# The opening of a one-core attention and two-MLP kernel: first state sums behind the first product, first outputs ahead of the second scores, few wide dummy products for many small ones

## The chip, the cores and the metric

The kernel runs on one core of a Trainium2 chip. The core has five engines with an instruction stream each: PE (TensorE, matmul), DVE (VectorE), ACT (ScalarE), POOL (GpSimd) and SP (SyncE, which here only issues DMAs). They meet through semaphores. The metric is the device time of one execution in microseconds, the median of three runs. PE has two clock levels, 1.2 and 2.4 GHz; the profile writes them as a granted clock of 0.50 and 1.00.

## The reference, cut to what matters

```
# attention, B=4 H=8 S=768 D=48, a state of D x D per head:
y[t]  = r[t] . (state + (u*k[t]) v[t]^T)
state = w[t][:, None] * state + k[t] v[t]^T
# x = y as 3072 tokens x 384, then two MLPs
h = x @ w_in (384 x 2048);  x = (h * clip(h+3,0,6)/6) @ w_out
x = x / rms(x) * rms_g;     out = (silu(x @ w_gate) * (x @ w_val)) @ w_out2   (384 x 1536)
```

All inputs and outputs are float32.

## The kernel before

The sequence is cut into groups of 64 steps of two batches each; 24 groups `g` in all, groups 0 and 1 being the first 64 steps of the two pairs of batches. For a group, DVE scans the decays (`prep_scan`, tile `cum`), takes four reciprocals (`prep_inv`) and multiplies by the keys (`prep_k`, tile `ki`); POOL multiplies `r` by the decays (`prep_r`, tile `rd`) and, for groups 0 and 1 alone, `r` by `k` (`rk_mul`, tile `xo`). PE then forms the scores (`scores`), the transposed keys (`keys`), the state sums (`sums`) and the outputs (`outputs`, whose parts are `inside` and `inside3`), and for groups 0 and 1 the bonus term (`bonuses`). ACT puts the bonus on the diagonal (`fill_bonus`), copies the transposed keys (`copy_keys`, tile `kiT`) and rounds the outputs to the MLP's input (`x1_hi`, tile `xs`); DVE masks the scores (`mask_scores`), subtracts the rounded part (`x1_lo`) and takes the sums into the state (`update_state`).

The first MLP follows tile by tile, `e` = 0 to 6. Tile 0 is half a tile (256 tokens) and is made of groups 0 and 1; while it runs, groups 2 and 3 are worked in between. For each slice `f` of 16, PE makes the hidden product `up(e, f)` (three products per 128 rows, from a rounded weight and its rest), ACT and DVE apply the gate (`up_gate`, `hidden`), and PE adds the slice into the output, `down(e, f-2)`. In tile 0 the weights are still on their way: SP and ACT load them (`load_up`, `load_dn`), ACT rounds them (`split_up`), and POOL subtracts (also `split_up`). PE's `up(0, f)` waits for POOL's part.

Nothing is scheduled by a program: the order of each engine is the order in which its code is written, and each engine waits in order. What stands ahead of the first product of tile 0 is the opening, about 22 us. In it PE also runs dummy products on a tile of ones (`busy`, L1278), 20 + 3 + 3 + 4 of them, 128 columns each. A float32 matmul stands in the trace as two matmul records and two weight loads, so a dummy is four instructions.

## Time and profile before

| | us |
|---|---|
| median of 3 runs | 932.94 (931.34 to 935.17) |
| the profiled execution, its own time | 935.66 |
| its span | 933.9 |
| PE busy | 921.6 (99%) |
| DVE, ACT, POOL busy | 521.3, 361.7, 291.9 |

The span is what the trace covers; 1.8 us of the execution lie around it. PE is busy in nearly all of it, so the time is the sum of PE's work and of the few places where PE waits. Most of these lie in the opening. The trace's chain of waits goes back from the last instruction to what released each step; its pieces called "issue" are time in which an engine waited for nothing that the profile shows.

### The profile page before, as it was taken

What the parts mean: (1) busy time and instruction counts of PE and PEld (TensorE: products, weight loads), DVE (VectorE), ACT (ScalarE), POOL (GpSimd) and SP (SyncE); (2) the same over time, 40 slices, a digit from 0 to 9 for tenths busy, and PEclk for the clock granted to TensorE, in tenths of its full rate; (3) what the DMA queues carried; (4) which work ended last, traced back from release to release, by engine and by line L of the source; (5) the groups of instructions that cost most, each with busy time, mean ns of one, the idle gap of its engine ahead of it and who ended that gap; (6) DMA issues with size and microseconds to landing.
All of it is one profiled execution on the core that took longest, in us unless ns stands there. A gap on an engine that the chain in (4) does not pass through costs nothing.

```text
span 933.9 us, 17547 instructions
## 1 busy us (share of the span) xinstructions
PE 921.6 (99%) x7064; PEld 772.9 (83%) x7064; DVE 521.3 (56%) x752; ACT 361.7 (39%) x786; POOL 291.9 (31%) x244
## 2 busy tenths in 40 slices
PE   7999999999999999999999999999999999999998
PEld 7899988888888888888888888888888888888886
DVE  6888976566666666315774553553463373363332
ACT  4557454354444445336463123223223223223212
POOL 4789544454454444324351011011011001101000
PEclk9999999999999999999999999999999999999999
DMA  9874442233223231014221010010000001000000
GB/s 255 237 208 129 109 131 60 63 105 86 75 61 107 69 83 51 22 39 135 86 83 45 0 35 34 1 34 34 0 34 35 1 19 50 0 1 34 1 1 34
DMA packets 33008, 60.40 MB, mean 65 GB/s; under 512 B 6112, under 2 KB 19936, under 8 KB 32928
## 3 DMA queue, kind: packets, MB, share of 16 engines
q1 hardware_dynamic: 27104, 50.82, 18.7%
q10 hardware_dynamic: 5824, 8.47, 3.1%
q8 instruction: 56, 0.92, 0.4%
q14 instruction: 24, 0.20, 0.1%
HBM read 47.66 MB, written 9.44 MB: 61 GB/s over the span
## 4 chain that ended last, share of the span: by engine, by line
PE 93%; DVE 4%; issue 1%; DMA 1%; ACT 1%; SPq 1%; DVEq 0%; ACTq 0%
PE acc L1079 34%; PE bank L1050 11%; PE bank L1052 11%; PE bank L1051 11%; PE pair L1050 5%; PE pair L1051 5%; PE pair L1052 5%; DVE ki L731 1%; PE acc L1113 1%; PE pair L1132 1%; PE pair L1189 1%; PE pair L1161 1%; DVE cum L719 1%; PE bank L1068 1%; PE bank L1153 1%
## 5 line engine op out<-in xcount | busy, mean ns | idle before, releaser
L1079 PE MATMUL acc<-gs,w_dn 128*128 128x512 f32 (+1 forms) x1512 | 357.0, 382 | 1.2 <-issue 1.2
L1079 PEld LDWEIGHTS acc<-gs,w_dn 128*128 128x128 f32 x1512 | 272.9, 188 | 55.1 <-issue 1.3
L945 POOL TENSOR_TENSOR gs<-act_g,gs 128x512 fp32r<-128x512 f32 (+1 forms) x96 | 122.1, 1272 | 208.3 <-ACT gs L550 208.2
L1050 PE MATMUL bank<-xs,w_up 128*128 128x512 f32 (+1 forms) x459 | 171.9, 374 | 1.4 <-DVE state L762 1.2
L1052 PE MATMUL bank<-xs,w_up 128*128 128x512 f32 (+1 forms) x459 | 169.1, 368 | 0.0
L1051 PE MATMUL bank<-xs,w_up 128*128 128x512 f32 (+1 forms) x459 | 169.0, 368 | 0.0
L801 DVE SCALAR_TENSOR_TENSOR act_g<-act_u,bank 128x512 f32<-128x512 f32 (+1 forms) x112 | 67.5, 603 | 139.8 <-ACT act_u L542 139.8
L869 DVE TENSOR_TENSOR act_u<-act_u,bank 128x512 f32<-128x512 f32 x72 | 49.5, 688 | 146.8 <-ACT act_u L612 146.8
L542 ACT ACTIVATE act_u<-bank,half 128x512 f32<-128x512 f32 (+1 forms) x112 | 70.0, 625 | 150.8 <-PE bank L1052 139.9
L616 ACT ACTIVATE gs<-act_g 128x512 fp32r<-128x512 f32 x72 | 45.5, 632 | 155.9 <-DVE act_g L875 155.9
L1050 PEld LDWEIGHTS bank<-xs,w_up 128*128 128x128 f32 x459 | 86.4, 188 | 18.0 <-DVE state L762 1.6
L612 ACT ACTIVATE act_u<-bank 128x512 f32<-128x512 f32 x72 | 43.1, 598 | 149.0 <-PE bank L1052 149.0
L1051 PEld LDWEIGHTS bank<-xs,w_up 128*128 128x128 f32 x459 | 86.5, 188 | 14.8
L1052 PEld LDWEIGHTS bank<-xs,w_up 128*128 128x128 f32 x459 | 86.4, 188 | 14.6
L991 POOL TENSOR_TENSOR xs<-ntmp,xs 128x512 fp32r<-128x512 f32 x18 | 26.1, 1448 | 225.8 <-ACT xs L575 225.8
L731 DVE RECIPROCAL ki<-cum 112x128 f32<-112x128 f32 x96 | 84.2, 921 | 0.8
L550 ACT ACTIVATE gs<-act_g 128x512 fp32r<-128x512 f32 (+1 forms) x96 | 57.2, 596 | 69.4 <-DVE act_g L801 67.8
L875 DVE TENSOR_TENSOR act_g<-act_u,pair 128x512 f32<-128x512 f32 x72 | 49.5, 688 | 52.0 <-PE pair L1052 51.3
L879 DVE TENSOR_TENSOR gs<-act_g,gs 128x512 fp32r<-128x512 f32 x72 | 55.3, 768 | 36.8 <-ACT gs L616 36.3
L1050 PE MATMUL pair<-xs,w_up 128*128 128x512 f32 x144 | 56.0, 389 | 0.0
L1051 PE MATMUL pair<-xs,w_up 128*128 128x512 f32 x144 | 56.0, 389 | 0.0
L1052 PE MATMUL pair<-xs,w_up 128*128 128x512 f32 x144 | 56.0, 389 | 0.0
(121 smaller groups left out, 1121.6 us busy)
## 6 DMA issues: line engine op xcount, KB each, us to landing
rkn<-in_rkN SPq DMA_DIRECT2D x22, 384.0 KB, 4.1
rkt<-in_rkT SPq DMA_DIRECT2D x44, 192.0 KB, 3.6
val<-in_valN SPq DMA_DIRECT2D x22, 256.0 KB, 3.0
x<-x_dram SPq DMA_DIRECT2D x6, 768.0 KB, 4.2
dec<-in_decT SPq DMA_DIRECT2D x46, 97.5 KB, 2.3
x_dram<-xo SPq DMA_DIRECT2D x5, 768.0 KB, 4.1
out<-xo SPq DMA_DIRECT2D x5, 768.0 KB, 3.3
raw_dn<-in_w_out SPq DMA_DIRECT2D x14, 192.0 KB, 4.8
```

What stands on the lines that cost most here:

```text
L542: act.activation(act_u[:, f % 2, tok], ps_h[f % 2][:, tok], ACT.Relu, scale=1.0 / 6.0, bias=half[:, 0:1]).then_inc(s_u, 1)
L550: act.activation(gs[:, f % GRING, 0, tok], act_g[:, f % 2, tok], ACT.Copy).then_inc(s_ghi, 1)
L731: dve.reciprocal(ki[0:DP, q, p, :, :], cum[0:DP, q, p, :, 1:T1]).then_inc(s_inv, 1)
L801: dve.scalar_tensor_tensor(out=g_of(e, f), in0=act_u[:, f % 2, tok], scalar=1.0, in1=ps_h[f % 2][:, tok], op0=ALU.min, op1=ALU.mult).then_ ...
L869: dve.tensor_tensor(act_u[:, f % 2, :], act_u[:, f % 2, :], ps_h[f % 2][:, :], ALU.mult).then_inc(s_silu, 1)
L875: dve.tensor_tensor(act_g[:, f % 2, :], act_u[:, f % 2, :], ps_v[f % 2][:, :], ALU.mult).then_inc(s_h, 1)
L879: dve.tensor_tensor(gs[:, f % GRING, 1, :], act_g[:, f % 2, :], gs[:, f % GRING, 0, :].bitcast(F32), ALU.subtract).then_inc(s_hlo, 1)
L945: pool.tensor_tensor(gs[:, f % GRING, 1, tok], act_g[:, f % 2, tok], gs[:, f % GRING, 0, tok].bitcast(F32), ALU.subtract).then_inc(s_glo, 1)
L1050: pe.matmul(dst, w_hi, x_hi, start=first, stop=False)
L1051: pe.matmul(dst, w_hi, x_lo, start=False, stop=False)
L1052: last = pe.matmul(dst, w_lo, x_hi, start=False, stop=end)
L1079: last = pe.matmul(ps_o[m][:, tok], w[:, wp, m * P:(m + 1) * P], gs[:, f % GRING, xp, tok], start=f == 0 and a == 0, stop=f == nf - 1 and ...
```

## The change

- PE: `sums(0)` moves from ahead of `scores(1)` to behind the first hidden product `up(0, 0)`. `keys(1)` moves to behind `up(0, 2)`, into bank 7. `outputs(0)` now precedes `scores(1)`. The dummies become 4 + 1 + 2 of 512 columns.
- DVE: of group 1's reciprocals the last, and its `prep_k`, come behind `mask_scores(0)`. `update_state(0)` comes behind `hidden(0, 0)`.
- POOL: the wait for both scans stands ahead of `prep_r(0)` instead of `rk_mul(1)`.
- ACT: the fourth `load_up` and the two `load_dn` leave it for SP; `split_up(0)` and both `place_val3` come ahead of group 1's bonus; `keep_last` comes behind `x1_hi(1)`; `copy_keys(1)` comes behind `up_gate(0, 3)`.
- SP: group 2's `r` and `k` wait for `s_ki` 2 too, three slices of weights follow at once instead of two, and from slice 2 on the loop issues two slices a step.

```diff
         def key_bank(g):
-            return ps_h[g] if g < 2 else ps_c
+            return ps_h[0] if g == 0 else ps_c
...
+            sp.wait_ge(s_ki, 2)
             load_rk(2)
-            sp.wait_ge(s_ki, 2)
-            for f in range(FIRST_UP, FIRST_UP + 2):
+            for f in range(FIRST_UP - 1, FIRST_UP + 2):
                 load_up(sp, f)
-                load_dn(sp, f - 2)
+                load_dn(sp, f - FIRST_UP + 1)
             load_dec(3)
             load_rkn(3)
             load_rk(3)
+            load_dn(sp, 3)
             for s in range(NF1):
-                if s + FIRST_UP + 2 < NF1:
-                    load_up(sp, s + FIRST_UP + 2)
-                if s + FIRST_UP < NF1:
-                    load_dn(sp, s + FIRST_UP)
+                for f in (s,) if s < 2 else range(2 * s - 2, min(2 * s, NF1)):
+                    if f + FIRST_UP + 2 < NF1:
+                        load_up(sp, f + FIRST_UP + 2)
+                    if f + FIRST_UP < NF1:
+                        load_dn(sp, f + FIRST_UP)
...
@@ ACT
-            for f in range(FIRST_UP):
+            for f in range(FIRST_UP - 1):
                 load_up(act, f)
-                if f < 2:
-                    load_dn(act, f)
...
+            copy_bonus(0)
+            for part in range(2):
+                fill_bonus(0, part)
+            place_val3(0)
+            copy_keys(0)
+            place_val3(1)
+            split_up(0)
+            copy_bonus(1)
+            for part in range(2):
+                fill_bonus(1, part)
+            x1_hi(0, 0)
+            split_up(1)
+            x1_hi(1, 0)
...
             for f in range(NF1):
                 up_gate(0, f)
+                if f == 3:
+                    copy_keys(1)
@@ DVE
+            prep_scan(1)
+            prep_inv(1, 0)
+            prep_inv(1, 1, slice(0, 2))
             dve.wait_ge(const, NCONST)
-            for g in range(2):
-                mask_scores(g)
+            mask_scores(0)
+            prep_inv(1, 1, slice(2, 3))
+            prep_k(1)
+            mask_scores(1)
             for g in range(2):
                 x1_lo(g, 0)
-            update_state(0)
             for f in range(NF1):
                 hidden(0, f)
                 if f == 0:
+                    update_state(0)
                     prep_scan(2)
@@ POOL
             rk_mul(0)
+            pool.wait_ge(s_cum, 2)
             prep_r(0)
-            pool.wait_ge(s_cum, 2)
             rk_mul(1)
@@ PE
+                    if (e, f) == (0, 0):
+                        sums(0)
                     if (e, f) == (0, 2):
-                        sums_read(pe, 0)
+                        keys(1)
...
-                    pe.matmul(ps_o[0][:, 0:P], ones[:, :].bitcast(F32), ones[:, :].bitcast(F32), start=True, stop=True)
+                    pe.matmul(ps_c[:, :].rearrange("p (a c) -> p a c", c=P), ones[:, :].bitcast(F32),
+                              ones[:, :].bitcast(F32).unsqueeze(1).broadcast_to([P, 4, P]), start=True, stop=True)
             pe.wait_ge(s_ones, 1)
-            busy(20)
+            busy(4)
             bonuses(0)
-            busy(3)
+            busy(1)
             pe.wait_ge(const, NCONST)
             scores(0)
             keys(0)
-            busy(3)
             bonuses(1)
-            pe.wait_ge(s_bonus, 1)
-            sums(0)
-            busy(4)
+            busy(2)
+            outputs(0)
             scores(1)
-            outputs(0)
+            pe.wait_ge(s_bonus, PLACED)
             outputs(1)
-            pe.wait_ge(s_bonus, PLACED)
-            keys(1)
             run1(0, 0, half_a)
```

PE's order of the opening before (L1278 the dummies, L1177 `bonuses`, L1132 `scores`, L1142 `keys`; behind the last row come the sums of group 0, L1153):

```order
L1043 UNCONDITIONAL_BRANCH
L1278 MATMUL acc<-ones 128x128 x20
L1177 MATMUL acc<-u_h,xo 128x4 x4
L1278 MATMUL acc<-ones 128x128 x3
L1132 MATMUL pair<-rd,ki 64x64 x16
L1142 MATMUL bank<-ident,ki 128x112 x4
L1278 MATMUL acc<-ones 128x128 x3
L1177 MATMUL bank<-u_h,xo 128x4 x4
```

And now (the numbers of lines are four to six higher: L1284 the dummies, L1181, L1136, L1146 as above, L1165 and L1172 `inside` and `inside3`):

```order
L1049 UNCONDITIONAL_BRANCH
L1284 MATMUL bank<-ones 128x512 x4
L1181 MATMUL acc<-u_h,xo 128x4 x4
L1284 MATMUL bank<-ones 128x512
L1136 MATMUL pair<-rd,ki 64x64 x16
L1146 MATMUL bank<-ident,ki 128x112 x4
L1181 MATMUL bank<-u_h,xo 128x4 x4
L1284 MATMUL bank<-ones 128x512 x2
L1165 MATMUL pair<-att,val 64x64 x12
L1172 MATMUL pair<-att,val 64x64 x12
L1136 MATMUL acc<-rd,ki 64x64 x16
L1165 MATMUL acc<-att,val 64x64 x12
```

The outputs of group 0 (written to `pair`) now stand ahead of the scores of group 1 (written to `acc`); the 64 instructions of `sums(0)` and 23 of 30 dummies are gone from the opening.

DVE's order before, from group 0's keys to the first gate:

```order
L738 TENSOR_TENSOR ki<-rkt,ki 112x512
L719 SCALAR_TENSOR_TENSOR cum<-dec,first 112x520
L731 RECIPROCAL ki<-cum 112x128 x4
L738 TENSOR_TENSOR ki<-rkt,ki 112x512
L745 COPY_PREDICATED att<-mask,pair 128x512
L745 COPY_PREDICATED att<-mask,acc 128x512
L785 TENSOR_TENSOR xs<-pair,xs 128x2x3x64
L785 TENSOR_TENSOR xs<-acc,xs 128x2x3x64
L759 TENSOR_TENSOR state<-bank,last 112x4x48
L759 TENSOR_TENSOR state<-acc,last 112x4x48
L801 SCALAR_TENSOR_TENSOR act_g<-act_u,bank 128x256
```

And now:

```order
L740 TENSOR_TENSOR ki<-rkt,ki 112x512
L721 SCALAR_TENSOR_TENSOR cum<-dec,first 112x520
L733 RECIPROCAL ki<-cum 112x128 x3
L747 COPY_PREDICATED att<-mask,pair 128x512
L733 RECIPROCAL ki<-cum 112x128
L740 TENSOR_TENSOR ki<-rkt,ki 112x512
L747 COPY_PREDICATED att<-mask,acc 128x512
L787 TENSOR_TENSOR xs<-pair,xs 128x2x3x64
L787 TENSOR_TENSOR xs<-acc,xs 128x2x3x64
L803 SCALAR_TENSOR_TENSOR act_g<-act_u,bank 128x256
L761 TENSOR_TENSOR state<-bank,last 112x4x48
L761 TENSOR_TENSOR state<-acc,last 112x4x48
```

The first mask moved ahead of the fourth reciprocal of group 1, and the two state operations moved behind the first gate.

## Rows read from the trace of the kernel before

**Rows 1.** The page: busy time, share of the span, instructions.
```profile
PE 921.6 (99%) x7064; PEld 772.9 (83%) x7064; DVE 521.3 (56%) x752; ACT 361.7 (39%) x786; POOL 291.9 (31%) x244
```

**Rows 2.** Chain of waits, 0 to 36 us: start, length in us, what.
```profile
9.19 1.48 DVE ki L738
...
11.86 3.40 DVE ki L731 x4
15.35 0.70 DVE ki L738
...
17.71 2.75 issue
...
25.60 1.41 DVE cum L719
```

**Rows 3.** PE in order of time: start, us, instruction, records, [idle before <- releaser].
```profile
1.84 7.30 PE L1278 MATMUL acc<-ones 128*128 128x128 f32 x40 [1.84 <-DVE ones L886]
9.13 1.03 PE L1177 MATMUL acc<-u_h,xo 112*128 112x4 f32 x8
...
20.46 0.33 PE L1168 MATMUL pair<-att,val 64*64 64x64 f32 x4 [2.75 <-issue]
20.59 0.69 PE L1161 MATMUL acc<-att,val 64*64 64x64 f32 x24
...
22.66 1.62 PE L1068 MATMUL bank<-xs,w_up 128*128 128x256 f32 x6
```

**Rows 4.** DMA queues while PE stops, 17.4 to 17.8 us: packets, MB, share.
```profile
q8 instruction: 1, 0.02, 22.0%
```

**Rows 5.** Stretches: length, busy (records) by engine, PE clock, DMA share, GB/s.
```profile
17.70:20.46 2.76, 0.01 (x1) 0.00 (x0) 0.00 (x0) 0.30 (x1) 1.91 (x2) 1.00 0.99 286
20.90:24.30 3.40, 3.40 (x55) 3.16 (x47) 1.65 (x4) 2.34 (x5) 2.35 (x3) 0.50 1.00 261
10.70:14.10 3.40, 2.85 (x53) 2.50 (x51) 3.37 (x4) 2.69 (x10) 2.19 (x2) 1.00 1.08 359
0.00:17.71 17.71, 15.18 (x220) 14.29 (x221) 13.53 (x18) 8.87 (x33) 7.32 (x15) 1.00 0.94 246
20.40:88.10 67.70, 66.76 (x992) 61.19 (x992) 57.42 (x93) 41.55 (x122) 54.53 (x50) 0.97 0.72 206
```

**Rows 6.** Stretches of the dummies alone: length, PE and PEld busy (records), clock.
```profile
3.00:5.00 2.00, 2.00 (x12) 2.00 (x11) 1.00 1.07 258
7.50:8.80 1.30, 1.30 (x14) 1.30 (x13) 1.00 1.05 216
```

**Rows 7.** POOL, DVE and ACT in order of time.
```profile
7.72 1.27 POOL L960 TENSOR_TENSOR xo<-rkt 112x512 f32<-112x512 f32 x1 [4.43 <-DMA rkt<-in_rkT]
8.94 1.19 POOL L968 TENSOR_TENSOR rd<-rkt,cum 112x512 f32<-112x512 f32 x1
...
15.96 0.73 DVE L745 COPY_PREDICATED att<-mask,pair 128x512 f32<-128x512 int32 x1
...
22.02 0.49 ACT L531 ACTIVATE xs<-acc 128x384 fp32r<-128x384 f32 x1 [0.23 <-PE acc L1168]
22.89 0.54 ACT L522 ACTIVATE kiT<-bank 128x448 f32<-128x448 f32 x1 [0.37 <-PE bank L1142]
...
31.52 1.06 ACT L510 ACTIVATE att<-diag,bonus 128x64 f32<-128x64 f32 x4 [3.49 <-DVE bonus L775]
```

**Rows 8.** PE stretches: L1153 alone, 14 to 15 us; all of PE, 36 to 61.
```profile
14.00:15.00 1.00, 0.68 (x32) 0.56 (x32) 1.00 1.05 311
...
36.00:61.00 25.00, 25.00 (x394) 1.00 0.79 235
```

**Rows 9.** SP issuing the seventh slice; DMAs by tile with us to landing.
```profile
21.23 0.42 SPq L320 DMA_DIRECT2D raw_up<-in_w_in  x1
...
raw_up<-in_w_in SPq DMA_DIRECT2D x12, 192.0 KB, 4.6
```

**Rows 10.** Chain of waits, 80 to 92 us.
```profile
88.14 1.25 issue
```

More of the change, by code:

```diff
@@ L665, in _ @@
             act.wait_ge(const, NCONST)
-            for g in range(2):
-                copy_bonus(g)
-                for part in range(2):
-                    fill_bonus(g, part)
-                place_val3(g)
-                if g == 0:
-                    copy_keys(0)
+            copy_bonus(0)
[11 more added lines that the diff above has]
+            x1_hi(1, 0)
             for g in range(2):
                 keep_last(g)
-            for f in range(2):
-                split_up(f)
-            x1_hi(0, 0)
-            split_up(2)
-            x1_hi(1, 0)
-            copy_keys(1)
-            for f in range(3, FIRST_UP):
+            for f in range(2, FIRST_UP):
                 split_up(f)
@@ L721, in prep_scan, with prep_inv @@
                                        ALU.mult, ALU.add).then_inc(s_cum, 1)
-            def prep_inv(g, part):
+            def prep_inv(g, part, some=slice(0, PAIRS)):
                 q = slot(g)
@@ L729, in prep_inv @@
                     keys_taken(dve, p_kt, g - 2)
-                for p in ((0,), (1, 2, 3))[part]:
+                for p in ((0,), (1, 2, 3))[part][some]:
                     dve.reciprocal(ki[0:DP, q, p, :, :], cum[0:DP, q, p, :, 1:T1]).then_inc(s_inv, 1)
@@ L886, in _ @@
             dve.tensor_scalar(ones[:, :].rearrange("p (b t) -> p b t", b=PB), first1[:, 0, :, 1:T1], 0.0, 1.0, ALU.mult, ALU.add).then_inc(s_ones, 1)
-            for g in range(2):
-                prep_scan(g)
-                for part in range(2):
-                    prep_inv(g, part)
-                prep_k(g)
+            prep_scan(0)
+            for part in range(2):
+                prep_inv(0, part)
+            prep_k(0)
+            prep_scan(1)
+            prep_inv(1, 0)
+            prep_inv(1, 1, slice(0, 2))
             dve.wait_ge(const, NCONST)
-            for g in range(2):
-                mask_scores(g)
+            mask_scores(0)
+            prep_inv(1, 1, slice(2, 3))
+            prep_k(1)
+            mask_scores(1)
             for g in range(2):
                 x1_lo(g, 0)
-            update_state(0)
             for f in range(NF1):
@@ L1088, in up @@
                     pe.wait_ge(s_wloU, f + 1)
-                if (e, f) == (0, 1):
-                    pe.wait_ge(s_kiT, 2)
                 dst = ps_h[f % 2][:, tokens(e)]
@@ L1138, in keys @@
                 pe.wait_ge(s_ki, g + 1)
-                if g >= 2:
+                if g >= 1:
                     sums_read(pe, g - 1)
```

## The prediction

> **What bounds the kernel now.** I read the page's busy times first: PE is busy 921.6 us of a span of 933.9 [rows 1], so only places where PE waits, or work given to or taken from PE, can move the time. By stretch, PE is busy 25.00 of 25 us between 36 and 61 us [rows 8]: from 36 us on tile 0 is bound by PE, and whatever lead the opening wins is handed on there. The change edits what lies before that. So I read the chain of waits up to 36 us [rows 2]. Until 16 us it runs over DVE: the keys of group 0 (1.48 us), the scan, four reciprocals of group 1 (3.40) and its keys (0.70). Then PE stops at 17.71 for 2.75 us, and "issue" says that no semaphore held it. PE resumes in the middle of the first outputs, four records from their end [rows 3]. The first product of tile 0 starts at 22.66 [rows 3]. From 25.60 the chain is on DVE again, with the scan of group 2 [rows 2], and goes over ACT's bonus (from 31.52 [rows 7]) back to PE near 36 us.
>
> What is the stop? Just ahead of it, between 17.4 and 17.8 us, a 16 KB instruction transfer stands in the DMA queues (0.02 MB on q8) [rows 4], while the queues are full (share 0.99, 286 GB/s) [rows 5]. PE and PEld had run 220 + 221 records by then, and 992 + 992 between this stop and a second one [rows 5], 1.25 us at 88.14 [rows 10]. I read both as PE having run out of code. The two places are 1984 matmul and load instructions apart, plus PE's own waits, so the places go by the count of instructions and will move when the count does.
>
> The Trainium skill (Runtime: NRT & Kernel Launch, "Instruction fetch mechanics") says that code comes in blocks of 16 KiB or 256 instructions, fetched while the one before runs, and that this is mostly hidden. Block size and distance agree with the rows (8 x 256 = 2048); hidden it is not, 2.75 and 1.25 us are seen. By the page's "mostly hidden" the stops would simply not be there.
>
> The stop has a second price. PE does one record in 17.70 to 20.46, and from 20.90 to 24.30 the granted clock is 0.50, that is 1.2 GHz [rows 5]. The first six records of the first product took 1.62 us in it [rows 3].
>
> **The change part by part.** Times are of the profiled execution; it took 935.66 us, 2.72 above the median of the three runs.
>
> *The order on POOL and group 0's keys.* The keys took 1.48 us beside POOL's `prep_r(0)` (8.94 to 10.13) [rows 7] and 0.70 for group 1 with POOL idle [rows 2]. POOL now waits for the second scan, so the keys end at 9.19 + 0.70 = 9.89, 0.78 earlier; the scan (1.19: from 10.67 to 11.86 [rows 2]) ends at 11.1. In return `prep_r(0)` runs 11.1 to 12.3 (1.19), and `rk_mul(1)` 12.3 to 13.6 (1.27) [rows 7].
>
> The Trainium skill (SBUF — State Buffer, "SBUF: two separate sides") explains the 1.48: a DVE operation with two SBUF inputs and a GpSimd operation lock each other out for the whole instruction. That speaks against another edit: `split_up(0)` now comes ahead of group 1's bonus on ACT, so POOL's half of it (15.0 to 16.0) can stand in front of group 1's keys. By the rule they end near 16.7 instead of 16.0; PE asks for them at 17.1 (below), so the sum is the same.
>
> *DVE.* Reciprocals of group 1 start at 11.1; three of 0.85 (3.40 / 4) [rows 2] end at 13.65, mask 0 takes 0.73 [rows 7], to 14.4, the last reciprocal to 15.25, the keys to 16.0. This is the same instant as before (15.35 + 0.70); what DVE gained it gave to the mask.
>
> *PE.* `scores(0)` starts at 12.3 and takes about 0.6 (32 small records, at the rate of the sums' 0.68 [rows 8]), `keys(0)` half as much; `bonuses(1)` waits for `rk_mul(1)` and takes 13.6 to 14.6 (1.03 [rows 3]). The two wide dummies are worth eight small ones: the small ones give 14 records in 1.30 us late in the opening, and 12 in 2.00 early [rows 6], so 16 records' worth is 1.5 to 1.7 or about 2.7 to 3.2; I take 1.7, PE having worked just before, so to 16.3. `outputs(0)` takes about 0.9 (0.69 us for one of its two parts, partly overlapped [rows 3]), to 17.15; `scores(1)` 0.6, mask 1 0.73, `outputs(1)` 1.0, ACT's rounding 0.49 [rows 7], each with its handover of 0.1: the first product starts at 20.3. Before, 22.66. That is -2.3: the stop of 2.75 gone from here, less 0.4.
>
> The four wide dummies at the start cost nothing: before, 40 records ended at 9.14 [rows 3]; 16 small ones' worth end near 8.3, and the next work waits for POOL until 8.99 (7.72 + 1.27) [rows 7].
>
> *Behind the first product.* At 2.4 GHz its nine records take 1.1 us instead of 1.8. `sums(0)` adds 0.56 to 0.68 us of PE (32 records [rows 8]), formerly in the opening. Then `update_state(0)` (two of 0.35) stands ahead of DVE's scan of group 2: 20.3 + 1.1 + 0.6 = 22.0, an ACT gate and the DVE gate in the meantime (to 22.4), the state to 23.0. The scan starts at 23.0, against 25.60 [rows 2]: -2.6. `copy_keys(1)` (0.54, of which 0.4 counts since ACT's operations overlap) [rows 7] stood beside PE and now stands between two bonus parts on ACT, on which the chain runs from 31.5 on: +0.4. `keys(1)` on PE (0.4) falls into gaps that PE has before 36 us. Handed on at 36 us: -2.2. If the later gaps all stay, the bounds of this part are -1.2 (wide dummies and mask slower than read) and -3.3 (DVE's chain not the limit, the clock's gain whole).
>
> *Loads.* Six 192 KB loads are moved or bunched and group 2's `r`, `k` wait from 12.82 to 16.0. The queues so have an empty stretch before 16 us, and a queue behind it. The seventh slice was issued at 21.23 [rows 9]; now three loads more stand ahead of it, about 22.5, landing 4.6 to 5.4 later, near 27.5. ACT wants it at 25.3 and stops for it in order. But behind it ACT only has the bonus of group 2, for which it idled 3.49 us [rows 7]. I cost it at nothing; if that cover is gone, it costs up to 1 us.
>
> *Code.* In the opening 23 dummies go, 92 instructions (four each), and `sums(0)` (64) and `keys(1)` (8) move behind. The instruction count of the first stop (441 records) now falls in the middle of `sums(0)`: 4 x 7 dummies, bonuses 32, scores 128, `keys(0)` 8, outputs 192, first product 18 make 406, and 35 more are in the sums. The block's transfer is asked for 256 instructions earlier, which is now within `outputs(0)`, near 15.5 to 16.5 us, when the queues are near empty. It has until 21.7; before it started at about 17.5 and PE ran again at 20.46, three microseconds later. If it starts before 18.7 it costs nothing. I take 0; the other bound is 2.75.
>
> The second stop moves on by 92 instructions as well, out of `down` at 88 us; -1.25 if nothing replaces it. Some other place where PE takes 256 instructions in under 3 us may replace it: every group has such a burst of small products (scores, outputs, sums), and any of them can come to lie across a block by the shift. I take -0.6, bounds -1.25 and +1.0.
>
> **Sum.** -2.2 - 0.6 = -2.8 on 935.66, or 932.9 for a profiled execution. Since the profiled one was 2.72 above the median and a median run may lack part of the stops that I take out, I take -2.5 from 932.94: 930.4 us.
>
> **Rivals.**
>
> A, *the clock.* Between 9 and 14 us PE now has less to do: it idles about 0.7 us before the bonuses, 1.4 before `scores(0)`, and 19 dummies fewer fill the rest; it was busy 2.85 of 3.40 us in 10.70 to 14.10 [rows 5], and will be about 1.6. If 1.2 GHz is granted from 14 us, the two wide dummies, on the path, take 1.3 to 1.6 more, the rest of the opening 0.3, the first product 0.7: scan 2 starts at about 25.4 and with the later +0.4 nothing is left of the opening. For it: the clock fell after a stretch with little work. Against: that stretch had one record in 2.76 us, none here is so empty. Result: 932.5 (-0.6 from the second stop and rounding). The Trainium skill (TensorE: Matmul & The Clock Gate, "Part 1: The HAM clock gate") says that the clock is low by default and released by activity; it gives no case half busy, so it moves no number.
>
> B, *the stop moves with its block, and the kernel is slower.* Place: inside `sums(0)`. It decides if the transfer starts after about 18.7 us, as it did on full queues. Then PE, at 21.7, waits about 2.7 us; `update_state(0)` and the scan, which now stand behind the sums, start at 25.7 instead of 25.60; ACT's copy adds 0.4, and the products run at 1.2 GHz again, behind which DVE's next gates slip by up to 1. +0.5 to +1.5, and if a new stop also replaces the second: 934.0. For it: before, the transfer was late on full queues; against: its request falls into the empty stretch.
>
> C, *both stops gone and PE bound earlier.* -3.3 - 1.25 = -4.6 and what the rest of the order gives: 928.0. For it PE would have to be the limit before 36 us, where its own gaps and DVE's chain say otherwise.
>
> D, *the loads.* The slices bunched after 16 us come too late for ACT and, through POOL, for PE: -2.2 + 1 - 0.6, 931.1; inside my range.
>
> **How the numbers follow.** The forecast with D: 0.56. A: 0.13. B: 0.13. C: 0.18. Half a percent, 4.7 us, is about what a measurement of this kernel can tell from no change, so faster means under 928.3: C mostly (0.15) and the edge of the forecast (0.06), 0.21. Slower, over 937.6, needs B with a second mechanism such as late weights: 0.07. Within: 0.72. Range for 8 in 10: from 927.0, a little under C, to 934.4, a little over B. The forecast's own range is 928.8 to 932.
>
> **What would show it.** In the new trace: group 0's keys 0.7 us, not 1.48; `prep_r(0)` behind the second scan; the first product at 20.3 (19.5 to 21); no "issue" of over 1 us on PE before 22 us; clock 1.00 from 7 us through 25; scan 2 at 23.0; the state sums in one piece; the piece at 88 us gone. Wrong would be: dummies of over 2.5 us at 14.5 (A); an idle PE in the middle of the sums with a q8 transfer that began after 18.7 (B); ACT waiting for raw weights with PE idle behind (D); the scan at 23 but PE at 36 us no earlier, for a reason that I don't have.

## The result and the profile after

The changed kernel took 935.56 us (median of 13 runs, 933.44 to 936.82), the kernel before 932.90 in the same session (13 runs, 929.47 to 935.17): a ratio of 1.0023 [1.0014, 1.0033]. It is slower: by 2.7 us in the medians, by 2.1 in the ratio, which is worked out from all runs and isn't the quotient of the medians. Forecast were 930.4 and a range up to 934.4. Timed again in another session (e16 below) the ratio was 1.0026 [1.001, 1.0042]. The profiled execution took 936.48 us with a span of 934.7, only 0.8 over that of before, because the profiled execution of before was itself 2.7 above its median.

The page of the changed kernel (answers to [rows 1]: 46 records fewer, yet PE is busy 0.4 us longer):

```profile
PE 922.0 (99%) x7018; PEld 766.8 (82%) x7018; DVE 518.3 (55%) x752; ACT 361.5 (39%) x786; POOL 292.5 (31%) x244
```

Its chain of waits, 0 to 40 us (answers to [rows 2]):

```profile
10.87 1.82 issue
12.69 0.73 PE pair L1136 x32
...
24.27 8.44 DMA raw_up<-in_w_in
...
35.14 1.01 PE bank L1157 x26
36.15 2.78 PE acc L1117 x6
```

The stop of 2.75 us at 17.71 is gone, and so is that at 88 us. In their place stand an idle PE at 10.87, ahead of the first scores, and a load that lands 8.44 us after its issue. PE, in order of time (answers to [rows 3]):

```profile
9.77 1.11 PE L1284 MATMUL bank<-ones 128*128 128x512 f32 x2
12.69 0.69 PE L1136 MATMUL pair<-rd,ki 48*64 48x64 f32 x32 [1.82 <-issue]
...
14.88 3.63 PE L1284 MATMUL bank<-ones 128*128 128x512 f32 x4
18.44 0.58 PE L1165 MATMUL pair<-att,val 64*64 64x64 f32 x24
...
22.57 0.95 PE L1074 MATMUL bank<-xs,w_up 128*128 128x256 f32 x6 [0.75 <-ACT xs L533]
```

The first product starts at 22.57, not at 20.3 as forecast; before, it started at 22.66. The two wide dummies at 14.88 took 3.63 us. The stretches show why (columns as in [rows 5]):

```profile
11.42:14.83 3.41, 2.09 (x44) 1.87 (x45) 3.41 (x5) 2.04 (x9) 3.41 (x3) 1.00 0.81 252
14.83:18.25 3.42, 3.42 (x6) 1.21 (x5) 1.76 (x2) 2.59 (x11) 1.13 (x2) 0.50 0.16 31
...
31.90:35.30 3.40, 1.59 (x50) 1.35 (x53) 1.17 (x3) 2.57 (x8) 0.99 (x1) 1.00 1.11 299
35.30:38.70 3.40, 3.40 (x39) 2.86 (x34) 2.82 (x6) 2.05 (x8) 2.40 (x2) 0.50 1.02 268
```

The granted clock is 0.50, so 1.2 GHz, in 14.83 to 18.25 and again in 35.3 to 38.7, each time just behind a stretch in which PE was busy 2.09 and 1.59 us of 3.4. In the trace of before it was low only behind the stop for code. POOL, DVE and ACT (answers to [rows 7]):

```profile
11.41 1.17 POOL L974 TENSOR_TENSOR rd<-rkt,cum 112x512 f32<-112x512 f32 x1 [2.68 <-DVE cum L721]
...
15.16 0.99 POOL L938 TENSOR_TENSOR w_up<-raw_up,w_up 128x384 fp32r<-128x384 f32 x1 [0.19 <-ACT w_up L497]
...
24.09 1.01 POOL L958 TENSOR_TENSOR rkn<-rkn 128x384 f32<-128x384 f32 x1
25.18 1.02 POOL L960 TENSOR_TENSOR rkn<-rkn,u_b 128x384 f32<-128x384 f32 x1
```

```profile
9.49 0.69 DVE L740 TENSOR_TENSOR ki<-rkt,ki 112x512 f32<-112x512 f32 x1
10.10 1.23 DVE L721 TENSOR_TENSOR_SCAN cum<-dec,first 112x520 f32<-112x520 f32 x1
...
15.49 1.21 DVE L740 TENSOR_TENSOR ki<-rkt,ki 112x512 f32<-112x512 f32 x1
...
25.29 2.00 DVE L721 TENSOR_TENSOR_SCAN cum<-dec,first 112x520 f32<-112x520 f32 x1
```

```profile
32.73 0.52 ACT L497 ACTIVATE w_up<-raw_up 128x384 fp32r<-128x384 f32 x1 [4.55 <-DMA raw_up<-in_w_in]
33.16 1.05 ACT L512 ACTIVATE att<-diag,bonus 128x64 f32<-128x64 f32 x4
```

POOL's `prep_r(0)` waits 2.68 us for the second scan and ends at 12.58, and the first scores can't start before it: that is the idle PE. Scan 2 starts at 25.29 and takes 2.00 us instead of 1.41. ACT waits 4.55 us for the seventh slice; the bonus of group 2 stands behind it and starts at 33.16, 1.6 us later than before [rows 7], and `sums(1)`, which needs it, at 35.14.

One place further on shows what tile 0 hands on. The scores of group 3, in the kernel before and in the changed one:

```profile
46.84 0.69 PE L1132 MATMUL pair<-rd,ki 48*64 48x64 f32 x32
```

```profile
49.80 0.69 PE L1136 MATMUL pair<-rd,ki 48*64 48x64 f32 x32
```

The change stands 2.96 us behind at 47 us: `sums(1)` is 1.7 later (33.45 before), and the low clock from 35.3 on makes the other 1.3. The profiled execution of before then loses about 2.7 against it, in two places. At 88 us PE stops for code [rows 10]. At 100 us it waits for DVE, whose `update_state` (L762) frees the bank that the next product is written to; it ends at 100.04:

```profile
100.10 0.39 PE L1050 MATMUL bank<-xs,w_up 128*128 128x256 f32 x1 [0.89 <-DVE state L762]
```

```profile
99.43 0.61 DVE L762 TENSOR_TENSOR state<-bank,state 112x192 f32<-112x192 f32 x2
```

The changed one loses 0.8 ahead of tile 2; 0.8 is left at the end.

### The profile page after: what moved, and what is told of

The parts are those of the page before. It is cut to its first block, busy times and chain, and to the rows that moved or that the text cites. A ratio compares the mean times of both kernels' runs of the same rounds, so it can differ in the third digit from the quotient of the medians.

```text
span 934.7 us, 17454 instructions
## 1 busy us (share of the span) xinstructions
PE 922.0 (99%) x7018; PEld 766.8 (82%) x7018; DVE 518.3 (55%) x752; ACT 361.5 (39%) x786; POOL 292.5 (31%) x244
## 4 chain that ended last, share of the span: by engine, by line
PE 93%; DMA 2%; SPq 1%; DVE 1%; issue 1%; ACT 0%; POOL 0%; ACTq 0%; DVEq 0%; POOLq 0%
PE acc L1085 35%; PE bank L1056 11%; PE bank L1057 11%; PE bank L1058 11%; PE pair L1056 5%; PE pair L1057 5%; PE pair L1058 5%; PE acc L1117 2%; PE pair L1136 1%; PE pair L1193 1%; PE pair L1165 1%; PE bank L1157 1%; DMA raw_up<-in_w_in 1%; PE bank L1074 1%; SPq L383 1%
```

## The experiments

Each kernel ran beside the kernel before. "Low" is the mean time at 1.2 GHz in a run, worked out from the granted clock of all its runs (one minus the clock, times the span, times two); product and scores 3 are the starts, in the profiled execution, of the first product and of the scores of group 3; wait is what ACT then waits for the seventh slice. "Low" also counts a clock that falls behind PE's last matmul, where it costs nothing: the 1.1 us of low clock in e17's profile stand there.

| run | median / before | ratio | low | product | wait | scores 3 |
|---|---|---|---|---|---|---|
| before (session of e13) | 933.76 | 1 | 4.5 | 22.66 | 0 | 46.84 |
| changed | 935.56 / 932.90 | 1.0023 [1.0014, 1.0033] | 7.8 | 22.57 | 4.55 | 49.80 |
| e16_after_again | 936.75 / 933.76 | 1.0026 [1.001, 1.0042] | 8.6 | 24.55 | 0.21 | 49.57 |
| e1_loads_back | 937.11 / 933.81 | 1.0036 [1.0022, 1.005] | 10.0 | 24.30 | 0 | 50.23 |
| e2_fill | 935.14 / 933.81 | 1.0016 [1.0002, 1.0029] | 3.4 | 21.06 | 3.88 | 46.72 |
| e18_fill_again | 935.01 / 933.77 | 1.0011 [0.9997, 1.0026] | 3.7 | 20.80 | 4.27 | 48.72 |
| e17_fill_early | 933.91 / 933.77 | 1.0000 [0.9986, 1.0013] | 1.7 | 21.23 | 0.98 | 46.21 |
| e3_both | 932.75 / 933.81 | 0.9991 [0.9977, 1.0004] | 1.9 | 22.47 | 2.37 | 47.45 |
| e4_no_pair | 934.63 / 933.81 | 1.0007 [0.9995, 1.0019] | 12.1 | 19.99 | 4.32 | 47.05 |
| e5_small | 934.08 / 933.76 | 1.001 [0.9991, 1.0028] | 7.6 | 24.51 | 0 | 50.42 |
| e7_pool_back | 934.60 / 933.76 | 1.0009 [0.9996, 1.0023] | 5.4 | 21.28 | 3.34 | 47.10 |
| e14_after_early | 936.71 / 933.76 | 1.0022 [1.0007, 1.0037] | 8.1 | 25.43 | 0 | 50.39 |
| e9_sums_alone | 933.66 / 934.61 | 0.9991 [0.9977, 1.0004] | 6.4 | 21.23 | 0 | 46.28 |
| e12_loads_alone | 934.36 / 934.61 | 1.0006 [0.999, 1.0021] | 4.4 | 19.08 | 4.76 | 48.19 |
| e13_loads_early | 932.80 / 933.76 | 0.9993 [0.9979, 1.0007] | 1.6 | 19.38 | 0.25 | 43.57 |
| e6_before_wide | 932.46 / 933.76 | 0.9983 [0.9966, 0.9999] | 3.4 | 21.46 | 0.32 | 45.68 |
| e15_wide_early | 933.06 / 933.76 | 0.9989 [0.9978, 1.0] | 3.3 | 22.41 | 0 | 46.61 |
| e8_tuned | 932.87 / 933.76 | 0.9988 [0.9975, 1.0] | 2.4 | 20.20 | 0.33 | 45.16 |
| e10_tuned_small | 933.19 / 934.61 | 0.9987 [0.9976, 0.9998] | 3.4 | 21.04 | 0 | 46.96 |
| e11_wide_padded | 940.74 / 934.61 | 1.0067 [1.0051, 1.0084] | 2.8 | 30.79 | | |

**The clock and the loads, first as a square.** e1 is the changed kernel with the loads of before, e2 with the gap ahead of the first scores filled with two more wide dummies, e3 with both.

```diff
 # e1_loads_back (and e3_both): SP's loads, their waits and ACT's loads as before
-            for f in range(FIRST_UP - 1, FIRST_UP + 2):
+            for f in range(FIRST_UP, FIRST_UP + 2):
                 load_up(sp, f)
-                load_dn(sp, f - FIRST_UP + 1)
+                load_dn(sp, f - 2)
...
 # e2_fill (and e3_both): ahead of scores(0)
-            busy(1)
+            busy(3)
```

> The changed kernel with the weight loads of the kernel before (six early ones on ACT, group 2's r and k not held for the keys, one slice a step on SP). Theory L (loads): the wait of ACT for the seventh slice (4.55 us at 32.73 in the changed kernel) is what undoes the opening; here it is gone, the first state sums of group 1 start near 33.0 instead of 35.14, the clock does not fall to 0.50 at 35 us, and the time is 2 to 3 us under the changed kernel: 932.5 to 933.5. Theory O (the opening itself: dummies at 1.2 GHz, order on POOL and PE) as the only cause: the time stays within 1 us of the changed kernel's 935.6. The first product starts at 22.5 by both.

> The changed kernel with three wide dummies instead of one ahead of the first scores, so that PE works through most of the 2.4 us in which it idled. Theory C (clock): the clock stays at 1.00 from 8 us through 25, the two wide dummies at 14.9 take 1.8 us instead of 3.6, and the first product starts at 20.8 instead of 22.57. By theory L the time then moves by under 0.7 us (935.0 to 935.6), since the loads behind group 1's keys are where they were and ACT still waits for the seventh slice until about 32.7. If the opening alone is the cause, it moves by 1.8: 933.8. If the clock does not depend on this idle stretch, the first product stays at 22.5.

> Both edits: early loads as before, three wide dummies ahead of the first scores. By L and C together: first product at 20.8, no ACT wait, DVE's scan of group 2 near 23.5, 930.5 to 931.5, that is 4 to 5 us under the changed kernel and 1.5 to 2.5 under the kernel before. If L and C are not additive (the queues, full again, hold PE's code transfer, which stops PE inside the state sums): 932.5 to 934, with an idle PE of 1 to 3 us between 21 and 24.

The loads alone are not the cause: e1 is no faster than the changed kernel, and its clock is low from 14.39 for 6.8 us. The filled gap keeps the clock at 1.00 through the opening in e2's profile, and the dummies that took 3.63 us take 1.96:

```profile
9.85 2.82 PE L1284 MATMUL bank<-ones 128*128 128x512 f32 x6
12.87 0.69 PE L1136 MATMUL pair<-rd,ki 48*64 48x64 f32 x32 [0.20 <-issue]
...
15.04 1.96 PE L1284 MATMUL bank<-ones 128*128 128x512 f32 x4
```

But e2 is still 1.0016: with the first product at 21.06, ACT waits for the seventh slice.

```profile
30.55 0.53 ACT L497 ACTIVATE w_up<-raw_up 128x384 fp32r<-128x384 f32 x1 [3.88 <-DMA raw_up<-in_w_in]
```

With both edits (e3) the ratio is 0.9991. In its profile the clock fell at 10.46 already, under the dummies themselves, three of them taking 4.52 us, and the first scores waited for them until 14.55. That is not its usual run: six of its twelve show a clock of 1.000, and the profiled one took 1.4 us more than the median. ACT waited 2.37 us for the seventh slice here too, with the loads of before. By the ratios the loads of before are worth 2.3 us once the gap is filled (0.9991 for 1.0016) and nothing while it isn't (1.0036 for 1.0023 or 1.0026): the two causes don't simply add.

**The pair of dummies.** e4 is the changed kernel without the two wide dummies ahead of `outputs(0)`; e5 has four small ones for each wide one, which also adds 84 instructions.

```diff
 # e4_no_pair
-            busy(2)
 # e5_small
-            busy(4) ... busy(1) ... busy(2)      # 512 columns
+            busy(16) ... busy(4) ... busy(8)     # 128 columns
```

> The changed kernel without the two wide dummies behind group 1's bonuses. By theory C they cost 3.6 us of PE at 1.2 GHz, but the second scores still wait for group 1's keys (16.7), so the first outputs end by 16.2, the second scores start near 16.8 instead of 19.19 and the first product near 20.3 to 20.6, with the clock at 0.50 or 1.00. By theory L the time still moves by under 0.7 us: 935.0 to 935.6. If the opening alone is the cause: 933.5.

> The changed kernel with four small dummies for each wide one: the same columns, 84 PE instructions more. Theory W (the wide form itself makes the clock fall, since it has few instructions): the clock stays at 1.00 through 18 us and the pair behind the second bonuses takes 1.8 us instead of 3.6; the first product starts near 20.8. Theory C (idle time, whatever the form): it falls as in the changed kernel and the opening is the same within 0.4 us. Theory I (places go by the instruction count): PE's code transfers stand 84 instructions earlier in the program; the one that in the changed kernel began at 115.72, beside a slow SP issue (1.37 us at 115.71) ahead of the first product of tile 2, comes near 112.5, and that wait of PE falls from 1.28 to about 0.5 us. By C and I: 934.8; by W and I: 933.5 or less.

Without the pair the first product stands at 19.99, the earliest of this order, although the clock is low from 16.67 to 23.5. Over its runs the low time is 12.1 us, the longest of the table (7.8 and 8.6 with the pair), and the ratio, 1.0007, is still 1.5 to 1.8 us better than the changed kernel's, with intervals that overlap a little. So the pair keeps some of the clock and costs more on the path than that is worth. Four small dummies for each wide one take as long under the low clock (3.76 us at 15.99, as in e16 below), and it falls all the same, so the form makes no difference here. e5's ratio of 1.0010 goes with a second thing: it has no long wait ahead of tile 2, of which more below.

**The order on POOL.** e7 puts `prep_r(0)` ahead of the second scan again.

```diff
             rk_mul(0)
-            pool.wait_ge(s_cum, 2)
             prep_r(0)
+            pool.wait_ge(s_cum, 2)
             rk_mul(1)
```

> The changed kernel with POOL's order of before (r of group 0 ahead of the wait for the second scan). Group 0's keys take 1.48 again instead of 0.69, but the first scores start near 11.0 instead of 12.69, since group 0's r is there by then. Theory C: PE's idle stretch of 1.82 ahead of the first scores shrinks to under 0.4, the clock stays at 1.00 over the two wide dummies (1.8 us instead of 3.6), and the first product starts near 21; total 1 to 2 us under the changed kernel (933.5 to 934.5). If the idle time only moves (behind the keys of group 0, PE waiting for the second r times k), the clock falls as in the changed kernel: 935.6 again, which would leave the fall to idle time anywhere in the opening.

The first scores start at 10.62 and the gap goes behind the keys (1.03 us of idle PE ahead of 12.88, for `rk_mul(1)`); the clock falls at 15.11 for 3.4 us and again at 21.94. The dummies take 2.44 us, and the first product comes 1.3 us earlier than in the changed kernel's first profile. The ratio, 1.0009, is less than half of the loss, and the low time falls from 7.8 or 8.6 us to 5.4: POOL's wait is a good part of what starves PE, not all. How large a part, the intervals, which overlap, don't tell.

**The late slice, by itself.** e12 is the kernel before with only the loads of the change. e13, e14 and e17 take the lateness away: the two slices behind the sixth are issued ahead of group 3's decays, `r` and `k`.

```diff
 # e13 (on e12), e14 (on the changed kernel), e17 (on e2), e15 (on e6 with the new loads)
                 load_up(sp, f)
                 load_dn(sp, f - FIRST_UP + 1)
+            for f in range(FIRST_UP + 2, FIRST_UP + 4):
+                load_up(sp, f)
             load_dec(3)
...
-                    if f + FIRST_UP + 2 < NF1:
+                    if f >= 2 and f + FIRST_UP + 2 < NF1:
                         load_up(sp, f + FIRST_UP + 2)
```

> The kernel before with the changed kernel's placement of loads alone (three instead of six weight loads early on ACT, group 2's r and k and all later slices behind group 1's keys, two slices a step). Theory L: the queues run empty before 16 us, ACT waits for the seventh slice by 2 to 4 us near 28 to 32, group 1's first state sums start 1 to 2 us later than 33.45, and the time is 0.5 to 2 us over the kernel before. In its favour: PE's code for the first outputs comes through the empty queues, so the 2.75 us stop at 17.7 shrinks. If that outweighs the loads: the time is that of the kernel before or up to 1 us less.

> The kernel before with the changed kernel's loads (as e12), but the two slices of w_in behind the sixth (the seventh among them) are issued ahead of group 3's decays, r and k instead of behind them. Theory L (the late seventh slice gives the opening's lead back): the first product stays at about 19.1 us, ACT waits under 1.5 us for the seventh slice instead of 4.76, the clock doesn't fall at 31.6, the scores of group 3 stand at 46.0 or earlier (48.19 in e12, 46.84 before), and the time is 931 to 932.5 (0.997 to 0.9985 of before). Theory Q (the queues, not the order, are the limit): the wait moves to another load, group 3's or a later slice, scores of group 3 stay near 48 and the time near 934 (1.000).

The new loads alone take the stop for code out of the opening (its transfer starts at 14.45 instead of 17.54) and put the first product at 19.08, 3.6 us earlier. Then ACT, in e12 and in e13:

```profile
30.04 0.52 ACT L497 ACTIVATE w_up<-raw_up 128x384 fp32r<-128x384 f32 x1 [4.76 <-DMA raw_up<-in_w_in]
```

```profile
25.31 0.53 ACT L499 ACTIVATE w_up<-raw_up 128x384 fp32r<-128x384 f32 x1 [0.25 <-DMA raw_up<-in_w_in]
```

In e12 PE idles 2.98 us ahead of `sums(1)` at 32.38 and runs at 1.2 GHz from 31.59 on:

```profile
31.59:35.00 3.41, 2.62 (x36) 2.26 (x37) 2.26 (x5) 2.34 (x8) 1.26 (x2) 0.50 1.08 285
35.00:38.40 3.40, 3.40 (x14) 3.12 (x13) 1.74 (x4) 0.51 (x3) 2.94 (x3) 0.50 1.04 283
```

A lead of 3.6 us is a lag of 1.35 at the scores of group 3. In e13 neither happens, and the lead there is 3.3 us. This shows the mechanism. (The lateness moves on: ACT now waits 2.46 and 3.26 us for the ninth and the eleventh slice, but PE doesn't wait for these.) Of the total less is left, 0.9993 against 1.0006 with intervals that overlap. e13's profile loses time again in three places: PE stops for code at 46 and at 85 us, and at 96.68 it waits 0.54 us for DVE's `update_state`, as the kernel before did at 100.10.

```profile
46.26 0.43 PE L1191 MATMUL pair<-rd,state 48*48 48x64 f32 x13 [0.76 <-issue]
...
86.47 0.63 PE L1081 MATMUL acc<-gs,w_dn 128*128 128x256 f32 x4 [1.04 <-issue]
```

> The changed kernel, with the two slices behind the sixth issued ahead of group 3's loads. Theory L with the clock's fall as a second cause: the first product stays at about 22.5 (the fall in the opening isn't touched), ACT's wait for the seventh slice shrinks from 4.55 to under 1.5 us, sums(1) at about 33.5 instead of 35.1, no low clock from 35.3 on, 934 to 934.8 (1.000 to 1.001). Theory F (the idle PE and the clock alone decide): 935.5 as the changed kernel (1.0023).

> The changed kernel unchanged, once more beside the others. The first comparison gave 1.0023 [1.0014, 1.0033]; the same is expected, 935.6 to 936.8. In the profile: clock low from about 14.8 and from about 35.3 us, the two wide dummies over 3 us, ACT's wait for the seventh slice over 4 us. If it is the state of the queues in one execution that made these, they are missing here or stand elsewhere.

In the changed kernel the edit gave nothing (1.0022). In e14's profile the clock was low from 12.39 to 22.63 and the first product stood at 25.43, so late that no slice was missing. e16 shows the same of the changed kernel itself, run again; PE in this second profile:

```profile
13.13 0.69 PE L1136 MATMUL pair<-rd,ki 48*64 48x64 f32 x32 [2.13 <-POOL rd L974]
...
15.77 3.76 PE L1284 MATMUL bank<-ones 128*128 128x512 f32 x4
19.46 0.92 PE L1165 MATMUL pair<-att,val 64*64 64x64 f32 x24
```

The clock was low for 6.8 us from 14.79 and for 3.4 from 25.02; the first product came at 24.55, 2 us later than in the first profile, and the slice was in time. So the kernel pays one or the other: a longer stretch of low clock ahead of the first product, or the late slice and a low clock behind it. Both end at scores of group 3 near 49.7. With the gap open, early slices therefore have little to win. My expectation, that the late slice would stand in e16 as well, was wrong. The runs that were not profiled bear the clock out. In the session of e16:

| mean granted clock of the run | before | changed |
|---|---|---|
| 1.000 | 6 runs, median 931.33 | none |
| 0.998 | 17 runs, 933.76 | 2 runs, 934.14 |
| 0.996 and lower | 12 runs, 935.10 | 10 runs, 937.00 |

Over the changed kernel's 12 runs, time follows the low stretch with 0.46 us per us (correlation 0.92), near the half that a clock halved under full work would cost; over before's 35 it is 0.41 (0.63). By these slopes 4.1 us more at 1.2 GHz (8.6 against 4.5) make 1.7 to 1.9 of the 3.0 us between the medians. That is an estimate from runs that happened to differ, and the slope isn't the same everywhere: it is 0.28 to 0.50 in e1, e3, e4, e5, e9, e14 and e17, and under 0.1 in e2, e7, e12, e13 and e15.

> The changed kernel with three wide dummies ahead of the first scores (as e2_fill) and the two slices behind the sixth issued ahead of group 3's loads. Theory CL (the clock's fall, and where the clock is kept the late slice, give the gain back): first product at 20.5 to 21.5 us, clock 1.00 in the opening, ACT's wait for the seventh slice under 1.5 us instead of 3.88, scores of group 3 at 45.5 or earlier instead of 46.72, 932.5 to 933.5 (0.9985 to 0.9995 of before). Theory F (only the clock counts, and e2's remainder is something in the order of the work): as e18, 1.0016, 935.1.

> e2_fill unchanged, beside e17_fill_early: 1.0016 [1.0002, 1.0029] again, and a wait of ACT of over 3 us for the seventh slice wherever the first product stands ahead of 22 us.

e17 closes the square inside the changed kernel, with its loads, its POOL order and all: gap filled and slices early, 1.0000 [0.9986, 1.0013]. e18, the filled gap alone, again waits 4.27 us for the slice and takes 935.01, 1.1 us more. In its profile the clock was 1.00 up to 21.12, so through the dummies, and then fell for 3.4 us, and again at 34.78 behind the wait for the slice. By the ratios the filled gap is worth 0.7 to 1.4 us (from 1.0023 or 1.0026 to 1.0016 or 1.0011) and the early slices 1.0 to 1.5. The second is about what these runs resolve (the intervals overlap); it stands on the wait in the trace as well, which was 3.3 to 4.8 us in the six profiles of the table that had the change's loads as they are and a first product ahead of 22.6 (the changed kernel, e2, e4, e7, e12, e18), and under 1 us in e13 and e17, which have them early. Together the two edits take the loss away (1.0000 [0.9986, 1.0013] for 1.0023 [1.0014, 1.0033]); they don't bring the gain that was forecast.

**Parts that cost nothing.** e9 is the kernel before with `sums(0)`, `update_state(0)`, `keys(1)` and `copy_keys(1)` moved as in the change.

```diff
-            pe.wait_ge(s_bonus, 1)
-            sums(0)
...
                     if (e, f) == (0, 0):
+                        sums(0)
                     if (e, f) == (0, 2):
-                        sums_read(pe, 0)
+                        keys(1)
```

> The kernel before with the first state sums (and with them the state update, the transposed keys of group 1 and their copy) behind the first product; dummies, loads, POOL and the order of masks as before. Theory S (the moved sums cost by themselves, in DVE's chain and ACT's copy): the scan of group 2 starts about 1 us later behind the first product than before (3.5 instead of 2.9 us), and the time is 0.5 to 1.5 us over the kernel before. Theory N (they cost nothing): within 0.4 us of the kernel before, since PE has gaps until 36 us.

0.9991 [0.9977, 1.0004], with the first product 1.4 us earlier: the change's first named part costs nothing that shows. What I charged to ACT's copy (+0.4) is too little to be seen in such an interval.

**Better versions.** e6 is the kernel before with wide dummies (5, 1, 1, 1 for 20, 3, 3, 4); e8 the changed kernel with the loads of before, 5, 2 and 2 wide dummies and `split_up(0)` behind group 1's bonus; e10 is e8 with small dummies; e15 is e6 with the new loads and the early slices.

```diff
 # e6
-            busy(20) ... busy(3) ... busy(3) ... busy(4)     # 128 columns
+            busy(5) ... busy(1) ... busy(1) ... busy(1)      # 512 columns
 # e8
-            busy(4) ... busy(1)
+            busy(5) ... busy(2)
```

> The kernel before with wide dummies alone (5, 1, 1, 1 for 20, 3, 3, 4 small ones; 88 PE instructions fewer), nothing else changed. By theory W the clock falls in the opening and the time rises by 1 to 2 us over the kernel before. By theory C it stays at 1.00 until PE's stop, if there is one. By theory I PE's stop in the first outputs (2.75 us at 17.71) moves 88 instructions on, to the end of the second outputs, or goes since PE reaches it later; and the one at 88 us goes; then the time is that of the kernel before or up to 2 us less.

> Both edits of e3_both in milder form, and POOL kept off group 1's keys: loads as before, five wide dummies at the start (PE busy until the first bonuses) and two ahead of the first scores, split_up(0) behind group 1's bonus. Theories C and L: no fall of the clock before 25 us, the first scores at 12.8, group 1's keys 0.69 instead of 1.2 to 1.5, the first product at 20.8 to 21.2, 930.5 to 931.5. If full queues or the lost width of dummies matter more, 932.5 to 933, as e3_both.

> e8_tuned with four small dummies for each wide one: the same columns, 108 PE instructions more. Theory I: PE's code transfers stand 108 instructions earlier; the wait of PE ahead of tile 2 (1.87 us at 113.01 in e8_tuned, beside an SP issue that took over 0.85 us) falls to about 0.5 us, and the time by about 1.0: 931.5 to 932. Against: PE may stop for code inside the first or second outputs, where it takes 256 instructions in 3 us: then 933 to 934. If the positions of the code don't matter: 932.9 as e8_tuned.

> The kernel before with wide dummies as in e6 (5, 1, 1, 1), the new loads and the two slices early. If the gains of e6 (-1.7) and of the loads without their lateness (-2) add: 930 to 931.5 (0.996 to 0.9975). If both only take away the same wait, the stop for code in the opening: 932.5 (0.9985). Slower than before if the wide dummies, with no stop behind them, leave PE idle before the first scores and the clock falls ahead of the first product: 934.5.

All four stand a little under the kernel before, by 0.11 to 0.17%, at the edge of what can be told; they don't differ from each other, and the gains don't add. In e15 the opening's stop is back, in the same record as in e6, although the loads are those that had removed it in e12:

```profile
21.15 0.49 PE L1170 MATMUL acc<-att,val 64*64 64x64 f32 x8 [2.67 <-issue]
```

**A failed test.** e11 was to give e6 back its count of instructions with 23 dummies of 4 columns for one wide one.

```diff
-            busy(5)
+            for _ in range(23):
+                pe.matmul(ps_o[0][:, 0:4], ...)
+            busy(4)
```

> e6_before_wide with 23 dummies of 4 columns in place of the first wide one: the wide form is kept, and the number of PE instructions is that of the kernel before. Theory I: what e6_before_wide won over the kernel before (0.17%) came from the positions of the code; here PE stops at the same two places as in the kernel before (in the first outputs, at the 448th instruction record, and near 88 us) and the time is the kernel before's, within 0.6 us (933.4 to 934.4). Theory W2 (the wide form itself saves time): 932.5 as in e6_before_wide.

```profile
1.83 9.98 PE L1283 MATMUL acc<-ones 128*128 128x4 f32 x46 [1.83 <-DVE ones L886]
11.67 6.50 PE L1278 MATMUL acc<-ones 128*128 128x512 f32 x8
```

The tiny dummies took 217 ns a record and the wide ones behind them 0.85 us a record up to 16.9, so the first product came 9.3 us later than in e6. Its total says nothing on its question.

## Why the prediction was wrong, point by point

The steps that held: the keys of group 0 took 0.69 us (0.70 forecast) and ended within 0.3 of the forecast; the keys of group 1 ended at 16.7 as the rule on POOL said, at no cost to PE (SP's loads, which wait for them, do start 0.7 later for it); both stops for code went; the state sums moved at no cost that e9 could show.

**The step that failed** is the price of the two wide dummies ahead of `outputs(0)`: "I take 1.7, PE having worked just before". They took 3.63. The reason is rival A, given 0.13: PE was busy 2.09 of 3.41 us, and the clock fell at 14.83. For 10.70 to 14.10 I had estimated 1.6 us of work (it was 1.53) and dismissed it, since the only fall that before's trace showed followed an empty stretch. That was the wrong reading of one example: it bounds the case from one side only. The 1.9 us of it, and 0.4 for scores that started at 12.69 and not 12.3, are the 2.3 by which the first product missed (22.57 for 20.3). e2 confirms the cause (1.96 us for the pair with the gap filled), e4 that the pair stood on the path (19.99 without it), and e7 that POOL's wait, which I had costed only by what it saves DVE (0.78), is part of what starves PE.

**The loads** (rival D): "I cost it at nothing; if that cover is gone, it costs up to 1 us". I had the landing as 4.6 to 5.4 us after an issue at 22.5, near 27.5. It was issued at 24.27, behind all that SP had issued since 16.73, group 3's loads among it (one of these took 1.22 us, beside a transfer of code at 21.51), and landed 8.44 us later; its cover, ACT's idle time ahead of group 2's bonus, was gone by 1.6 us, and 1.3 more went to the low clock behind it. As D stood inside the forecast, the two were taken as alternatives; in the first profile they followed each other.

**What the two don't explain.** The median lies 5.2 us over the forecast. e17, which has the clock's fall and the late slice out of the way, gives back 2.1 to 2.4 of it and ends level with the kernel before, where 2.5 us of gain were forecast. 0.7 of that is the wait ahead of tile 2 (1.04 us in e17, 0.33 before). The rest stays open; the first candidate is the base of the sum, which took the stops of one profiled execution, itself 2.72 us above the median, for nearly a part of every run.

**Scan 2**: forecast at 23.0, it started at 25.29, which follows from the late first product, and took 2.00 us, beside POOL's two multiplications of `rkn` (24.09 to 26.20), against 1.23 with POOL idle at 10.10 and 1.41 for the same scan before. The Trainium skill (SBUF — State Buffer, "SBUF: two separate sides") says that a DVE instruction with two SBUF inputs and a GpSimd instruction that reads SBUF lock each other out for a whole instruction. The trace agrees: the scan ends 1.1 us behind POOL's multiplication. I had used the rule for the keys and not for the scan, 0.6 us on the path.

**Code**: -0.6 was taken for the second stop. It went in the trace (-1.25), and the wait ahead of tile 2 grew from 0.33 to 1.11 us, with an SP issue beside a transfer of code (last section). Rival C's condition, both stops gone, was met, and its 928.0 was still missed by 7.6, since what the stops covered came to the surface. How much of the stops of before lies in its median, I can't tell from one profile; it stays open.

**Two sums** don't come out as written: rival A's -0.6 on 932.94 gives 932.3, not 932.5, and C's -4.6 gives 928.3, not 928.0. Neither changes the account.

The chances: 0.07 for slower by over 0.5% fits, as the loss is 0.23%. But the range ended at 934.4 as if one mishap at most could happen, where A and D together stood open.

## What to carry to other kernels

A stop that is removed from an opening also removes the slack in which the other engines' waits hid: list what is late next, each with its margin, and add them up when one leads to the next. Work taken away from PE in a stretch where it waits for others can halve its clock, and the next thing on its path is then paid twice; fill the gap where PE waits, not behind it, and never with work that ends later than the data arrives. A single example of a clock fall tells that it can fall, not when it does not.

## What the runs showed of the hardware that I had not expected

- **The clock falls without an empty stretch, and not each time.** It fell behind 2.09 of 3.41 us busy (changed kernel), behind 1.59 of 3.40, and in e7 behind 2.38 of 3.41, with no idle time of over 1.9 us in any of them. In the changed kernel's first profile, in e2's and in e17's it stayed at 1.00 behind the stretch just ahead of the first product, with 1.59 to 1.60 of 3.40 us busy; in e18's it fell there, at 21.12, in the very order of e2. So one profile doesn't tell whether an order keeps its clock; the low time over all its runs tells more.
- **PE's stops for code sit at fixed counts.** I count PE's matmul, load and wait records (448 are 440 or 441 without the waits). Up to tile 2, every stop of over 0.8 us, start to start, that no semaphore explains stood behind record 448 (before 2.97 us, e6 2.33, e9 1.77, e10 0.86, e11 2.80, e15 2.88), 1216 (e13 0.97), 2496 (before 1.53, e13 1.32) or 2752 (e4 0.86): at 448 and then 3, 8 and 9 times 256 further on. The waits at 100.10 in before and at 96.68 in e13 are no such stops, as a semaphore of DVE ends them; both stand some 10 us behind the stop at 2496, and whether they come from it isn't tested. Record 448 cost nothing in the changed kernel (e16 too), e1 to e5, e7, e8, e12 to e14, e17 and e18. From the start of the transfer to PE's next record it took 2.4 to 3.0 us. The Trainium skill (Runtime: NRT & Kernel Launch, "Instruction fetch mechanics") calls the cost of crossing such a block mostly hidden; here up to 3.0 us were seen.
- **A DMA issue on SP is slow beside a transfer of code.** Nine in ten issues take 0.3 to 0.6 us in before. In the changed kernel's profile, ahead of tile 2 (two issues, 2.00 us together, 1.37 of it the second), and the queues in 115.5 to 116.5 us:

```profile
115.08 2.00 SPq L383 DMA_DIRECT2D xs<-y  x2
```

```profile
q8 instruction: 1, 0.02, 6.4%
```

  In before, 13 issues were over 0.85 us, and all 13 lay within 1 us of the start of a transfer of code, where 58 of all 324 issues lay; in the changed kernel 12 of 13, in e12 11 of 11, in e17 15 of 15. PE's idle time ahead of tile 2 was 1.0 to 1.7 us in the changed kernel, e1 to e4, e6 to e8, e14 and e16 to e18, and 0.8 in e15; it was 0.33 or 0.34 in before, e5 and e9 to e13. Small dummies for wide ones, which change little but the count of instructions, took it away both times (e5 from the changed kernel, e10 from e8). Whether the transfer slows the issue or both are slowed by a third thing, the runs don't tell.
- **Tiny dummies aren't cheap.** At the start of the kernel 4 columns cost 217 ns a record (46 records in 9.98 us), more than 128 columns did (40 records in 7.30 us [rows 3], 183 ns).
